# Attention scores stored with the queries in another order, and early loads dealt out anew

## The reference

```python
f = 1.0 / (1.0 + np.exp(-f_logit))
for t in range(S):
    state = f[:, :, t, :, None] * state + np.einsum('bhd,bhe->bhde', k[:, :, t], v[:, :, t])
    y[:, :, t] = np.einsum('bhd,bhde->bhe', q[:, :, t], state)
# x: the heads of y side by side, 3072 tokens x 384
h = x @ w_in
g = np.where(h > 0.0, h, np.exp(np.minimum(h, 0.0)) - 1.0)
x = g @ w_out
h = np.maximum(x @ moe2_w_in, 0.0)
out = h * h @ moe2_w_out
```

## Time and profile before

| what | value |
|---|---|
| median of 3 runs | 971.96 us (971.29 to 976.01) |
| the profiled execution, its own time | 971.56 us |
| its span, first to last instruction | 969.8 us |
| PE busy | 951.4 us, 98% of the span |
| DVE, ACT, POOL busy | 504.0, 402.8, 236.8 us |

### The profile page before, as it was taken

How to read it: one execution, slowest core, us unless ns; L and a number is a source line. 1 busy time by engine, 2 the same in 40 slices (tenths; PEclk the granted TensorE clock), 3 DMA queues, 4 the chain that set the end, 5 groups by cost and what they waited for, 6 DMA issues and landing times.

```text
span 969.8 us, 27529 instructions
## 1 busy us (share of the span) xinstructions
PE 951.4 (98%) x11636; PEld 785.4 (81%) x11636; DVE 504.0 (52%) x746; ACT 402.8 (42%) x706; POOL 236.8 (24%) x193
## 2 busy tenths in 40 slices
PE   6899999999999999999999999999999999999998
PEld 5778787887887888888878888888888888888897
DVE  7788577576666656572326653343343433433432
ACT  4656545353534543453444452242332422423322
POOL 3102216354545445454424550000000000000000
PEclk6789999999999999999999999999999999999999
DMA  7552312212121211110203331002020030020100
GB/s 238 164 158 91 110 50 86 79 45 79 56 79 45 71 63 57 46 67 3 66 2 122 98 102 37 1 14 53 0 54 11 0 64 1 9 56 0 21 14 33
DMA packets 72428, 56.88 MB, mean 59 GB/s; under 512 B 37249, under 2 KB 64641, under 8 KB 72321
## 3 DMA queue, kind: packets, MB, share of 16 engines
q1 hardware_dynamic: 69472, 43.87, 16.6%
q10 hardware_dynamic: 2848, 11.44, 3.3%
HBM read 45.84 MB, written 9.44 MB: 57 GB/s over the span
## 4 chain that ended last, share of the span: by engine, by line
PE 97%; DMA 1%; DVE 1%; issue 1%; ACT 0%; SPq 0%; DVEq 0%
PE ps L1667 8%; PE ps L1663 8%; PE ps L1662 8%; PE ps L1137 8%; PE ps L1686 7%; PE ps L1682 7%; PE ps L1683 7%; PE ps L1276 6%; PE ps L1299 6%; PE ps L1278 6%; PE ps L1285 6%; PE ps L1301 6%; PE ps L1305 5%; PE ps L1206 2%; PE ps L1172 1%; PE ps L1154 1%
## 5 line engine op out<-in xcount | busy, mean ns | idle before, releaser
L1607 DVE TENSOR_TENSOR g<-g 128x512 f32<-128x512 f32 x96 | 66.8, 696 | 240.9 <-ACT g L1522 240.3
L1522 ACT ACTIVATE g<-ps 128x512 f32<-128x512 f32 x112 | 67.0, 598 | 276.9 <-PE ps L1667 272.6
L688 POOL TENSOR_TENSOR glo<-g,ghi 128x512 fp32r<-128x512 f32 x65 | 89.6, 1379 | 194.3 <-ACT ghi L513 194.3
L1662 PE MATMUL ps<-xhi,wts 128*128 128x512 f32 x336 | 130.9, 390 | 0.0
L1663 PE MATMUL ps<-xhi,wts 128*128 128x512 f32 x336 | 130.9, 390 | 0.0
L872 DVE SCALAR_TENSOR_TENSOR g<-e,g 128x512 f32<-128x512 f32 x80 | 57.8, 723 | 136.7 <-ACT g L507 136.7
L1682 PE MATMUL ps<-ghi,wts 128*128 128x512 f32 x294 | 114.4, 389 | 0.0
L1683 PE MATMUL ps<-ghi,wts 128*128 128x512 f32 x294 | 114.4, 389 | 0.0
L506 ACT ACTIVATE e<-ps 128x512 f32<-128x512 f32 x80 | 47.8, 598 | 158.7 <-PE ps L1285 158.7
L1276 PE MATMUL ps<-xhi,wts 128*128 128x512 f32 x240 | 98.9, 412 | 0.2 <-ACT g L507 0.2
L1278 PE MATMUL ps<-xhi,wts 128*128 128x512 f32 x240 | 94.7, 395 | 0.3 <-issue 0.3
(11 more groups left out here) (132 smaller groups left out, 1555.8 us busy)
## 6 DMA issues: line engine op xcount, KB each, us to landing
raw<-w SPq DMA_DIRECT2D x52, 192.0 KB, 2.4
q<-qk SPq DMA_DIRECT2D x22, 256.0 KB, 3.7
gate<-fl SPq DMA_DIRECT2D x10, 512.0 KB, 4.4
k<-qk SPq DMA_DIRECT2D x10, 512.0 KB, 3.7
x<-xo ACTq DMA_DIRECT2D x6, 768.0 KB, 3.3
xs<-x ACTq DMA_DIRECT2D x6, 768.0 KB, 4.4
v<-vn SPq DMA_DIRECT2D x11, 384.0 KB, 3.6
krow<-vn SPq DMA_DIRECT2D x20, 192.0 KB, 4.5
```

The source lines that it names most:

```text
L688: nc.gpsimd.tensor_tensor(out=glo[:, f % 2, :], in0=g[:, f % 2, :], in1=ghi[:, f % 2, :].bitcast(F32), op=ALU.subtract).then_inc(s_glo, 1)
L1662: nc.tensor.matmul(h, w(0, k), xhi[:, k, :], start=(k == 0), stop=False)
```

## The change

The queries of a half (64) are stored in another order. Query t = 16 f + n, with f from 0 to 3, goes to place 4 n + f. The bits of the index are turned by two, so level l writes runs of `run(l)` = 4, 8, 16, 32, 1, 2 elements for l = 0 to 5, where it was 1, 2, 4, 8, 16, 32. To get there, `product` reads the moving operand (the queries) with a step of 16 elements between neighbours (32 at level 4) and still writes PSUM contiguously. `values` reads `PT` with a step of 4 elements and writes y in the true order. The masks are built in the new order by ten ACT instructions instead of four, and the gates of unit (0, 1) are activated between them. `take4` and `take5` write with steps.

In SP's list the loads are dealt out anew: the queries of (1, 0) and chunks 0 and 1 of w1 earlier, the gates of (1, 1) one wait later, the other chunks in other groups and after other waits, and the keys of (1, 0) last. In ACT's list `take4(0, 0)` stands before `pad_v(0, 0)`, and only chunk 4 is split between `krow_copy(0, 0)` and `krow_copy(0, 1)`, where three were. DVE's splits move likewise: six of its twelve now stand after `state_update(0, 1)`, where four did. On PE `last_column(0, 0)` moves ahead of `values(0, 1, 0)`.

```diff
@@ -195,6 +198,10 @@
+    def run(l):
+        return 1 << (l + 2) % 6
@@ -379,25 +386,24 @@
-        sp.wait_ge(*level(s_mm, 0, 0, 1))
+        load_q(1, 0)
+        load_weights(range(2))
+        sp.wait_ge(*level(s_mm, 0, 1, 1))
         load_gates(1, 1)
-        load_weights(range(1))
-        sp.wait_ge(*level(s_mm, 0, 0, 2))
-        load_q(1, 0)
-        sp.wait_ge(*level(s_mm, 0, 1, 1))
-        load_weights(range(1, 2))
         load_staged_v(0, 0)
-        sp.wait_ge(*level(s_mm, 0, 0, 4))
+        sp.wait_ge(*level(s_mm, 0, 1, 2))
         load_staged_v(0, 1)
         load_v(0, 0)
-        sp.wait_ge(*level(s_mm, 0, 0, 5))
-        load_weights(range(2, 4))
-        sp.wait_ge(*level(s_mm, 0, 0, 6))
+        sp.wait_ge(*level(s_mm, 0, 1, 3))
+        load_weights(range(2, 5))
+        sp.wait_ge(*level(s_mm, 0, 1, 4))
         load_v(0, 1)
+        load_weights(range(5, 8))
+        sp.wait_ge(s_kT, 1)
+        load_weights(range(8, 11))
+        sp.wait_ge(s_y, 1)
+        load_weights(range(11, STAGED))
         load_k(1, 0)
-        load_weights(range(4, 6))
-        sp.wait_ge(s_y, 1)
-        load_weights(range(6, STAGED))
@@ -425,11 +431,11 @@
-            data = level_pair(c, h, 4)[:, :, 0:X * 32].rearrange("p j (x t) -> p j x t", x=X)
+            data = level_pair(c, h, 4)[:, :, 0:X * 32].rearrange("p j (n two) -> p j n two", two=2)
+            there = scores(h).rearrange("p j x t -> p j (x t)").rearrange("p j (n four) -> p j n four", four=4)
             for n in range(4):
                 rows, at = slice(32 * n, 32 * n + 16), n % 2
-                last = nc.scalar.activation(scores(h)[rows, :, :, 32 * at + 16:32 * at + 32],
-                                            data[rows, :, :, 16 * at:16 * at + 16], ACT.Copy)
+                last = nc.scalar.activation(there[rows, :, :, 2 * at + 1], data[rows, :, :, at], ACT.Copy)
@@ -449,10 +455,11 @@
-            data = level_pair(c, h, 5)[:, :, 0:X * 32].rearrange("p j (x t) -> p j x t", x=X)
+            data = level_pair(c, h, 5)[:, :, 0:X * 32].rearrange("p j (n w) -> p j n w", w=2)
+            there = scores(h).rearrange("p j x t -> p j (x t)").rearrange("p j (n two w) -> p j n two w", two=2, w=2)
             for half in range(2):
                 rows = slice(HP * half, HP * half + 32)
-                nc.scalar.activation(scores(h)[rows, :, :, 32:64], data[rows], ACT.Copy).then_inc(s_ev5, 1)
+                nc.scalar.activation(there[rows, :, :, 1, :], data[rows], ACT.Copy).then_inc(s_ev5, 1)
@@ -615,22 +622,24 @@
-        for levels in (slice(0, 1), slice(1, MASKED)):
+        for levels in (range(1), range(1, 2), range(2, MASKED)):
+            if MASKED - 1 in levels:
+                gates(0, 1, True)
             for half in range(2):
                 rows = slice(HP * half, HP * half + HP)
-                n = levels.stop - levels.start
-                nc.scalar.activation(
-                    mask[rows, levels, :].rearrange("p l (x t) -> p l x t", x=X),
-                    mask_words[rows].rearrange("p (l i x t) -> p l i x t", l=MASKED, i=2, x=1)[:, levels, half, :, :]
-                    .to_broadcast([HP, n, X, 32]), ACT.Copy).then_inc(s_mask, 1)
-        gates(0, 1, True)
+                for l in levels:
+                    f = 4 if l < EARLY else 2
+                    last = nc.scalar.activation(
+                        mask[rows, l, :].rearrange("p (x n f) -> p x n f", x=X, f=f),
+                        mask_words[rows].rearrange("p (l i x f n) -> p l i x n f", l=MASKED, i=2, x=1, f=f)[:, l, half, :, :, :]
+                        .to_broadcast([HP, X, 32 // f, f]), ACT.Copy)
+                last.then_inc(s_mask, 1)
         gates(1, 0, True)
+        split_weights(range(0, 2))
         gates(1, 1, True)
-        split_weights(range(0, 1))
         nc.scalar.activation(warm[:, 1:2], warm[:, 0:1], ACT.Exp)
-        split_weights(range(1, 2))
+        take4(0, 0)
         pad_v(0, 0)
-        take4(0, 0)
@@ -639,9 +648,9 @@
-        split_weights(range(4, 7))
+        split_weights(range(4, 5))
         krow_copy(0, 1)
-        split_weights(range(7, STAGED))
+        split_weights(range(5, STAGED))
@@ -817,10 +826,10 @@
-            if l < 2 and not past(c, h, 2):
+            if l < 3 and not past(c, h, 2):
                 dve.wait_ge(s_mask, 2 * l + 2)
                 dve.wait_ge(s_zero, 2)
-            w = 1 << l
+            w = run(l)
@@ -1064,13 +1073,13 @@
-        split_weights(range(1))
+        split_weights(range(2))
         own_k_update(0, 1, 6)
-        split_weights(range(1, 4))
+        split_weights(range(2, 4))
         state_update(0, 0)
-        split_weights(range(4, 8))
+        split_weights(range(4, 6))
         state_update(0, 1)
-        split_weights(range(8, STAGED))
+        split_weights(range(6, STAGED))
@@ -1128,12 +1137,19 @@
-                        there = q_all[rows, at, HP * z:HP * z + HP].rearrange("p (n two w) -> p n two w", two=2, w=w)[:, :, 1, :]
-                        to = banks[half:half + m, j, x * 32:x * 32 + 32].rearrange("p (n w) -> p n w", w=w)
+                        block, to = q_all[rows, at, HP * z:HP * z + HP], banks[half:half + m, j, x * 32:x * 32 + 32]
                     else:
                         m = HP
-                        there = q_all[rows, at, HP:C]
-                        to = banks[half:half + m, j, a * HP:a * HP + HP]
+                        block, to = q_all[rows, at, HP:C], banks[half:half + m, j, a * HP:a * HP + HP]
+                    if l < EARLY:
+                        there = block.rearrange("p (f n two w) -> p two n w f", f=4, two=2, w=w)[:, 1, :, :, :]
+                        to = to.rearrange("p (n w f) -> p n w f", w=w, f=4)
+                    elif l < 6:
+                        there = (block.rearrange("p (f two n) -> p two n f", f=2, two=2)[:, 1, :, :] if l == 4 else
+                                 block.rearrange("p (two f n) -> p two n f", f=2, two=2)[:, 1, :, :])
+                        to = to.rearrange("p (n f) -> p n f", f=2)
+                    else:
+                        there, to = block.rearrange("p (f n) -> p n f", f=4), to.rearrange("p (n f) -> p n f", f=4)
@@ -1195,6 +1211,15 @@
+        def keys_blocks(rows, h, z, own, far):
+            if z:
+                return PT[rows, h % 2, own, :].rearrange("p (n f) -> p f n", f=4)
+            return PT[rows, h % 2, own:far + 1:far - own, :].rearrange("p z (n f) -> p z f n", f=4)
+        def y_columns(at, z):
+            return at.rearrange("p (f n) -> p f n", f=4) if z else at.rearrange("p (z f n) -> p z f n", z=2, f=4)
@@ -1202,9 +1227,9 @@
-                        blocks = PT[rows, h % 2, own:far + 1:far - own, :] if z == 0 else PT[rows, h % 2, own, :]
+                        blocks = keys_blocks(rows, h, z, own, far)
                         last = nc.tensor.matmul(
-                            pair(c, h, "Y")[32 * group:32 * group + 32, u, m * CELL + HP * z:m * CELL + C],
+                            y_columns(pair(c, h, "Y")[32 * group:32 * group + 32, u, m * CELL + HP * z:m * CELL + C], z),
@@ -1222,9 +1247,9 @@
-                        blocks = PT[rows, h % 2, own:far + 1:far - own, :] if z == 0 else PT[rows, h % 2, own, :]
+                        blocks = keys_blocks(rows, h, z, own, far)
                         last = nc.tensor.matmul(
-                            pair(c, h, "Y")[at:at + n, u, m * CELL + HP * z:m * CELL + C],
+                            y_columns(pair(c, h, "Y")[at:at + n, u, m * CELL + HP * z:m * CELL + C], z),
@@ -1403,8 +1428,8 @@
+        last_column(0, 0)
         values(0, 1, 0)
-        last_column(0, 0)
```

## The result

The changed kernel takes 994.01 us (991.59 to 995.77, 4 runs) against 971.94 for the kernel before, a ratio of 1.0219 with a 95% interval from 1.0200 to 1.0238. It is 22 us slower. The prediction of 970.2 us and its range to 979 missed it; the rival "PE reads slower" had put 995 on it and a chance of 17%.

What follows compares the result with a forecast made beforehand. PE's own instructions bound the kernel after the start; in the first 60 us the lists of DVE, ACT and SP can. Savings of 0.7 (takes) and 0.7 us (loads and lists) make 1.4, giving 970.2 us, range 966.0 to 979.0.

Steps and rivals of the forecast that it cites:

- PE reads slower: Rival: the step makes PE's stream of queries or `PT` slower than instruction issue; 25 us more, 995 us, chance 17%.
- The strided reads of PE: PE's stepped fp32 reads in the level products and `values`: cost bounded between nothing and 92 us, taken as nothing.
- The takes: DVE's copies of levels 0 and 1 at the start shed 0.6 us each, of which 0.7 us comes through.
- ACT's strided takes: `take4` and `take5` on ACT at the start: cost at most about 1.5 us, taken as nothing.
- The loads and the lists: At the start `krow_copy(0, 1)` runs from 39.4 us and `new_state(0, 1)` moves from 42.63 to 41.9: 0.7 us saved.
- the clock stays up: Rival: PE's clock may not fall after 46 us, so `hidden(1, 0)` runs faster; 1.8 us more saved, 968.4 us, chance 17%.

## Why the prediction was wrong

**The step that failed** is "The strided reads of PE", with "I take the lower end, nothing". The runs showed the rival that it names. Permuting in PSUM took 20.5 of the 22 us away. I had read the slow pace of fp32 (1.0 ns a column against 0.45) as room for a slow read. But that pace was one matmul's, while the code lays eight tiles of `values` side by side on the array, and 14.5 ns an instruction with 128 columns (0.11 ns a column) was already a pace by columns. A row that I had in hand said so: two halves with the same count of instructions, 0.93 and 0.80 us, differ only in columns. The Trainium skill's rule (SBUF — State Buffer, Specifications (TRN2)), which I weighed and set aside, was right in its sign and in its threshold. It names no price; half the rate was my reading of it, and the group with 128 columns took 2.0 times as long.

**The rival's 25 us were near, its terms were not.** That 995 came so near the measured 994 is in part luck. The first half of `values` doubled as written, but it counts in ten units and not in twelve: in the first two it grew as well and was made up for at the start. Its second half cost 0.36 us a unit where I had 0.13, level 6 cost 0.42 where I had under 0.1, and the six other levels 0.3 to 0.5 in sum (0.34 in the chain, (8.6 - 3.8) / 10 by the times) where I had nearly 1. Levels with few columns for each instruction pay little.

**The takes** were right: 0.72 us for levels 0 and 1, 1.32 for level 4 from chunk 2 on, and PE's wait of 1.15 us gone. Timeline of DVE after the change, with levels 0, 4 and 1:

```profile
201.46 0.72 DVE L837 COPY_PREDICATED PT<-mask,ps 128x512 f32<-128x512 uint8 x1
...
202.67 1.32 DVE L837 COPY_PREDICATED PT<-mask,ps 128x512 f32<-128x512 uint8 x1
...
210.90 0.71 DVE L837 COPY_PREDICATED PT<-mask,ps 128x512 f32<-128x512 uint8 x1
```

What they bring in time was not measured alone. The version with PSUM and old lists ends 0.9 us above the kernel before although it carries ACT's takes, which alone cost 2.2; so they would bring something near 1, if the two add. But prices at the start don't add: the version with PSUM and new lists carries takes (2.2 alone) and lists (1.9 alone) and ends 0.5 us above, which by the same sum would give the shorter takes 3.6. What they bring stays open.

**ACT's strided takes** were taken at nothing with a bound of 1.5 us. Alone they cost 2.2 us (1.3 to 3.2), in part with the clock that rose later in that run. The bound by DVE's ratio, 0.69 us an instruction, was close to the 0.63 measured; what I overrated was the slack, since I looked at unit (0, 0) and the chain goes through `take4(0, 1)`.

**The loads and the lists** were to bring 0.7 us. By their ratios the lists alone cost 1.9 (0.8 to 3.0), the loads alone 1.6 (0.3 to 2.8), and `krow_copy` earlier shows no gain. With the new order the new lists cost nothing that shows, read in SBUF with the step or written to PSUM with it, so this price holds for the old order only; and part of it may be the clock, which rose 3 us later there. I had checked when each load lands and not what it does to PE's pauses, though a pause of 1.22 us stood in the chain that I read the earlier trace rows. The masks had no price in the prediction: their ten instructions take 5.8 us of ACT, where the four took 2.9. And at the start the strided reads cost too: with the permuting in PSUM and all else as in the change, `hidden(1, 0)` starts at 53.35 us instead of 54.76. The other 3.4 of the 4.8 us are masks, takes, lists and clock together; no run splits them further.

**The clock.** In the profile of the changed kernel the matmuls of `hidden(1, 0)` still follow each other at 0.43 us, at a granted clock of 0.50 from 55 to 58 us, so the rival "the clock stays up" did not come true there. With the order alone they start 0.23 us apart at 54.25 us, so it can happen, but it gives back less than the order costs.

**Sum.** 20.6 us in ten units and 4.8 at the start are 25.4, against 24.2 between the two spans; the 1.2 too much were not traced.

## What to carry to other kernels

Where a layout has to be permuted and PE is the bound, let PE write PSUM with the step and read SBUF side by side: here the same permutation cost 20.5 us on one side and nothing that could be measured on the other. Before calling a strided read free, look at whether columns or instructions set the pace of that group, by comparing two groups with equal counts and unequal columns. And at a start that is full of loads, an earlier load isn't free because it lands in time: compare PE's pauses and waits before and after, in more than one profile, and don't add up prices that were measured one at a time.

## What the runs showed of the hardware

- PE's fp32 reads from SBUF: steps of 2 elements cost 0.04 us in 0.93 (ratio 1.0003), steps of 4 double a group with 128 columns an instruction (0.93 to 1.87 us) and lengthen one with 64 (0.80 to 1.16), and a step of 16 in level 6 takes a piece from 1.48 to 1.90. At half clock the step of 16 costs nothing (1.6 us both times).
- PE's fp32 writes to PSUM with a step of 16 elements cost nothing that shows (0.93 and 1.48 us as without, ratio 1.0005).
- ACT's copy from PSUM to SBUF with a read step of 2 and a write step of 4 takes 633 ns instead of 372 for 256 elements; written in runs of 2 from a read side by side, 621 instead of 583 for 512.
- DVE's `copy_predicated` on 512 elements takes 0.70 to 0.72 us with runs of 4 or more and 1.3 with runs of 1 or 2, whichever level has them.
- In the profile of the changed kernel the granted clock is given as 1.00 from the start to 54 us (0.97 over the first 60), while the eight transposes at 36.89 us take 1.94 us. In the kernel before they take 1.97 at a granted clock of 0.50, and 1.02 later on. From 55 to 58 us the profile gives 0.50, and matmuls of 512 columns follow each other at 0.43 us, so there the two agree. Early in a profile the spacing of like matmuls is the safer reading.
